# One attention and MLP kernel: the first score in two halves of its queries, head B's first row values by products with a unit matrix, and another order of the first two pairs

## What is computed

```python
# q, k, v: (4 batches, 8 heads, 576 positions, 64), f32
q_rot, k_rot = (rotate(q), rotate(k))          # [x1 cos - x2 sin, x1 sin + x2 cos]
scores = scale * np.matmul(q_rot, k_rot.transpose(0, 1, 3, 2))
scores = scores - np.max(scores, axis=-1, keepdims=True)
attn = np.exp(scores)
attn = attn / (np.sum(attn, axis=-1, keepdims=True) + 1e-09)
attn_out = np.matmul(attn, v)
# then, on the 2304 x 512 result: h = x @ w_in; solu = h * softmax(h);
# layer norm without bias times g_ln; @ w_out
```

## Time and profile before

| what | value |
|---|---|
| median of 3 runs | 488.84 us (488.19 to 488.97) |
| the profiled execution | 488.11 us, with a span of 486.3 us |
| granted TensorE clock | 1.00 of full speed |
| first maximum of pair 0 on PE | 11.29 us |
| first score of pair 0, of pair 1, of pair 2 | 16.13, 35.02, 52.46 us |

### The profile page before, as it was taken

How to read it: one execution, slowest core, us unless ns; L and a number is a source line. 1 busy time by engine, 2 the same in 40 slices (tenths; PEclk the granted TensorE clock), 3 DMA queues, 4 the chain that set the end, 5 groups by cost and what they waited for, 6 DMA issues and landing times.

```text
span 486.3 us, 7544 instructions
## 1 busy us (share of the span) xinstructions
PE 479.3 (99%) x2499; PEld 402.9 (83%) x2499; DVE 362.5 (75%) x566; ACT 255.3 (52%) x383; POOL 178.6 (37%) x208
## 2 busy tenths in 40 slices
PE   8899999999999999999999999999999999999997
PEld 8677888888888888888888878888888888888885
DVE  6767776787778678767866456999897899888731
ACT  4667777777677778777776353033223222322221
POOL 6855246426434642554361012343343121122110
PEclk9999999999999999999999999999999999999999
DMA  8503544545454544545423112233333233322232
GB/s 296 184 10 75 152 145 126 168 125 168 102 158 144 156 132 127 168 111 171 138 74 98 33 39 46 40 66 85 85 68 83 40 62 66 82 55 59 61 76 86
DMA packets 101006, 50.57 MB, mean 104 GB/s; under 512 B 90280, under 2 KB 90280, under 8 KB 99048
## 3 DMA queue, kind: packets, MB, share of 16 engines
q1 hardware_dynamic: 100152, 50.00, 38.1%
q10 hardware_dynamic: 816, 0.10, 0.1%
HBM read 33.33 MB, written 4.79 MB: 78 GB/s over the span
## 4 chain that ended last, share of the span: by engine, by line
PE 95%; DVE 2%; ACT 1%; DMA 1%; issue 0%; SPq 0%; DVEq 0%; ACTq 0%
PE ps L1022 25%; PE ps L1036 20%; PE ps L1050 20%; PE ps L989 18%; PE ps L960 8%; PE ps L1004 4%; DMA X<-x_in 1%; DVE X L681 1%; DVE nm L740 0%; ACT p_main L553 0%; DVE X L686 0%; ACT QK L509 0%; ACT QK L524 0%; DVE QK L715 0%; DVE KB L725 0%
## 5 line engine op out<-in xcount | busy, mean ns | idle before, releaser
L740 DVE TENSOR_REDUCE nm<-ps 128x1 fp32r<-128x576 f32 x144 | 108.0, 755 | 56.0 <-PE ps L960 54.0
L1022 PE MATMUL ps<-p_main,V 128*128 128x288 f32 x512 | 145.3, 406 | 0.0
L553 ACT ACTIVATE p_main<-ps 128x576 f32<-128x576 f32 x128 | 83.2, 650 | 47.0 <-PE ps L989 45.5
L1022 PEld LDWEIGHTS ps<-p_main,V 128*128 128x128 f32 x512 | 90.0, 190 | 13.7 <-ACT p_main L553 0.2
L381 POOL TENSOR_TENSOR X<-X,rope 128x1152 f32<-128x1152 f32 x26 | 68.3, 2643 | 89.2 <-DVE w_lo L757 89.0
L989 PE MATMUL ps<-QK 128*128 128x288 f32 x320 | 95.7, 380 | 0.8 <-ACT p_main L553 0.5
L1036 PE MATMUL ps<-w_hi,KB 128*128 128x512 f32 x288 | 91.5, 390 | 0.0
L1050 PE MATMUL ps<-w_hi,QK 128*128 128x512 f32 x288 | 91.0, 389 | 0.0
L989 PEld LDWEIGHTS ps<-QK 128*128 128x128 f32 x320 | 57.6, 189 | 20.8 <-issue 5.7
L989 PE MATMUL ps<-KB 128*128 128x288 f32 x320 | 67.8, 293 | 0.0
L574 ACT ACTIVATE X<-ps,neg_max 128x1024 f32<-128x1024 f32 x18 | 20.1, 1118 | 83.4 <-DVE neg_max L778 83.4
(11 more groups left out here) (88 smaller groups left out, 580.2 us busy)
## 6 DMA issues: line engine op xcount, KB each, us to landing
X<-x_in SPq DMA_DIRECT2D x13, 1152.0 KB, 5.1
V<-oe SPq DMA_DIRECT2D x213, 32.0 KB, 1.9
V<-v_in SPq DMA_DIRECT2D x32, 160.0 KB, 2.7
out<-X SPq DMA_DIRECT2D x18, 256.0 KB, 2.3
w_raw<-w_in SPq DMA_DIRECT2D x16, 256.0 KB, 2.9
xT<-x_in SPq DMA_DIRECT2D x2, 1152.0 KB, 10.3
xT<-oe SPq DMA_DIRECT2D x16, 144.0 KB, 2.4
inv<-inv_rows SPq DMA_DIRECT2D x16, 144.0 KB, 2.9
```

The costliest lines, as they stand in the source:

```text
L553: nc.scalar.activation(dst[:, :].rearrange("p (b c) -> p b c", b=2), score_ps[:, :, 0:HALF], ACT.Exp, scale=SCALE).then_inc(exp_done, 1)
L740: nc.vector.tensor_reduce(nm[g][:, at:at + 1], src[:, :, 0:HALF], AX_XY, ALU.max, negate=True)\
L1022: ins = nc.tensor.matmul(o_ps[a][:, half, 0:HALF], v, p[:, half * HALF:(half + 1) * HALF], start=(k == 0), stop=(k == 9))
```

## The change

Four things are edited:

- `score(0, 0)` and `score(0, 1)` are replaced by `half_score(s, half)`, each for 288 of the queries. The exponential of score 0 is taken in two instructions, one for each half. Row values 0 to 2 (`FRONT`) are copied to `KB` first, and the first half score stands ahead of the last row product.
- Head B's row values of pair 0 come from four products with the unit matrix (`first_row_b`) and one copy on ACT; DVE's transposition and SP's four DMAs for them go.
- The maxima of pair 1 begin at step 4 of pair 0 (before: step 3), those of pair 2 at step 1 of pair 1 (before: step 0), and `max_slot` gives the last six of pair 1 the banks 4, 5 and 0, 1 in turn.
- ACT's and DVE's work for pairs 1 and 2 is written at other steps; the second copy of pair 1's queries of head A moves from ACT (`second_queries(1, 0)`) to DVE.

```diff
-FIRST_MAXIMA = [((), (), ()), ((), (), ()), ((), (), ()), ((), (), (0,)), ((1,), (), (2,)), ((3,), (), (4,)),
-                ((), (5,), ()), ((6,), (), (7,)), ((), (8,), ())]
-SECOND_MAXIMA = [((), (), (0,)), ((), (1,), ())] + [((s,), (), ()) for s in range(2, STEPS)]
+FIRST_MAXIMA = [((), (), ())] * 4 + [((), (), (0,)), ((1,), (), (2,)), ((3,), (4,), ()), ((5,), (), (6,)), ((7,), (), (8,))]
+SECOND_MAXIMA = [((), (), ()), ((0,), (), (1,)), ((), (2,), ())] + [((s,), (), ()) for s in range(3, STEPS)]
...
-            if k < STEPS + SPARE:
-                return max_ps[2 * ((k - STEPS) % 2)], k - 1
+            if STEPS + SPARE <= k < 2 * STEPS:
+                return max_ps[(k - STEPS) % 2], k - 1
             return max_ps[0], k
...
-            sp.wait_ge(kb_ones[0], 2)
-            rows_of_b(0)
...
             act.wait_ge(kb_ones[0], 2)
-            act.wait_ge(first_rows, BOTH)
-            nc.scalar.activation(KB[0][D:D + 1, 1, 0:MAIN], ps[0:1, 2, 0:MAIN], ACT.Copy).then_inc(first_rows_set, 1)
+            act.wait_ge(first_rows, FRONT)
+            nc.scalar.activation(KB[0][D:D + 1, 1, 0:FRONT * P], ps[0:1, 3, 0:FRONT * P], ACT.Copy).then_inc(first_rows_set, 1)
             act.wait_ge(first_rows, BOTH + 1)
...
+            act.wait_ge(half_scored, 1)
+            nc.scalar.activation(p_main[0][:, 0:HALF], score_ps[:, 0, 0:HALF], ACT.Exp, scale=SCALE).then_inc(half_done, 1)
+            act.wait_ge(score_ready, 1)
+            nc.scalar.activation(p_main[0][:, HALF:S], score_ps[:, 1, 0:HALF], ACT.Exp, scale=SCALE).then_inc(exp_done, 1)
...
                         if s == 2:
+                            act.wait_ge(first_rows_b, BOTH)
+                            nc.scalar.activation(KB[0][0:1, 1, S + 2 * TAIL:WIDE], ps[0:1, 0, 0:MAIN], ACT.Copy)\
+                              .then_inc(first_rows_b_set, 1)
+                        if s == 3:
                             high(1, 0)
-                            second_queries(1, 0)
...
+            dve.wait_ge(rot_done, 2)
+            nc.vector.tensor_copy(QK[1][other(0), 0, 0:S], x_of(1)[own(0), 1, :]).then_inc(second_set, 1)
             low_keys(1, 0)
...
-                if s == 5:
-                    third_keys()
-                if s == 6:
-                    third_queries()
+                    if s == 7 and place == 0:
+                        third_keys()
+                        third_queries()
...
+            def first_row_b(j):
+
+                pe.wait_ge(max_taken, max(BOTH + j + 2, STEPS - 2))
+                nc.tensor.matmul(ps[0:1, 0, j * P:j * P + P], nm[1][:, j:j + 1], ident_r[:, :], start=True, stop=True)\
+                  .then_inc(first_rows_b, 1)
...
+            def half_score(s, half):
+
+                for k, (keys, queries) in enumerate(((QK[0][:, 1, :], QK[0][:, 0, :]), (KB[0][:, 0, :], KB[0][:, 1, :]))):
+                    ins = nc.tensor.matmul(score_ps[:, half, 0:HALF], keys[:, s * P:s * P + P],
+                                           queries[:, half * HALF:(half + 1) * HALF], start=(k == 0), stop=(k == 1))
+                return ins
...
             for i in range(3):
                 row_scores(0, i)
-            for j in range(BOTH):
+            for j in range(FRONT):
                 first_row(j)
                 row_scores(0, j + 3)
+            first_row(FRONT)
+            row_scores(0, STEPS - 3)
+            pe.wait_ge(low_q_done[0], 1)
+            pe.wait_ge(copy_done[0], 1)
+            pe.wait_ge(kb_ones[0], 2)
+            half_score(0, 0).then_inc(half_scored, 1)
             first_row(BOTH)
+            pe.wait_ge(first_rows_set, 3)
+            half_score(0, 1).then_inc(score_ready, 1)
             row_scores(0, STEPS - 2)
+            pe.wait_ge(half_done, 1)
+            half_score(1, 0)
+            row_scores(0, STEPS - 1)
+            pe.wait_ge(exp_done, 1)
+            half_score(1, 1).then_inc(score_ready, 1)
```

More of the change, by code:

```diff
@@ L231, in max_slot, with hi_set @@
                 return max_ps[k % 3], k - 2
-            if k < STEPS + SPARE:
-                return max_ps[2 * ((k - STEPS) % 2)], k - 1
+            if STEPS + SPARE <= k < 2 * STEPS:
+                return max_ps[(k - STEPS) % 2], k - 1
             return max_ps[0], k
+        def hi_set(m, a, copies):
+            by_vector = a == 0 and (m >= 2 or (m == 1 and copies == 2))
+            return 2 * m + copies - int(by_vector)
         def fronts(t):
@@ L610, in _ @@
                 for s in range(STEPS):
[L611 to L615, removed]
+                    if n or s:
+                        exp(n, s)
                     if n == 0:
                         if s == 2:
+                            act.wait_ge(first_rows_b, BOTH)
+                            nc.scalar.activation(KB[0][0:1, 1, S + 2 * TAIL:WIDE], ps[0:1, 0, 0:MAIN], ACT.Copy)\
+                              .then_inc(first_rows_b_set, 1)
+                        if s == 3:
                             high(1, 0)
-                            second_queries(1, 0)
-                        if s == 3:
+                        if s == 4:
                             high(1, 1)
-                        if s == 4:
+                        if s == 5:
                             second_queries(1, 1)
@@ L628, in _ @@
                             act.wait_ge(gain_loaded, 16)
+                        if s == 8:
+                            high(2, 0)
+                    elif n == 1:
+                        if s == 0:
+                            second_queries(2, 0)
+                        if s == 1:
+                            high(2, 1)
+                        if s == 2:
+                            take_o(0, 1)
+                        if s == 3:
+                            second_queries(2, 1)
+                        if s == 4:
+                            add_eps(0)
+                            w_high(0)
                     else:
-                        if s == 0 and 2 <= n < PAIRS - 1:
+                        if s == 0 and n < PAIRS - 1:
                             second_queries(n + 1, 1)
@@ L733, in row_max @@
                     dve.wait_ge(first_rows, BOTH + 1)
+                if i == BOTH + 1 and m == 1:
+                    dve.wait_ge(first_rows_b, BOTH)
                 if i == 0 and m >= 2:
                     dve.wait_ge(turned[0], m - 1)
-                if i == BOTH + 1 and m >= 1:
-                    dve.wait_ge(turned[1], m)
+                if i == BOTH + 1 and m >= 2:
+                    dve.wait_ge(turned[1], m - 1)
                 src = max_slot(k)[0]
@@ L741, in row_max @@
                   .then_inc(max_taken, 1)
-                if (i == BOTH and m >= 1) or i == STEPS - 1:
+                if m >= 1 and (i == BOTH or i == STEPS - 1):
                     dve.wait_ge(max_taken, k + 1)
@@ L947, in row_scores @@
                     pe.wait_ge(max_taken, ahead)
+                if k == STEPS:
+                    pe.wait_ge(first_rows_b_set, 1)
+                if k == STEPS + SPARE:
+                    pe.wait_ge(o_taken, 1)
                 if i == BOTH and m >= 1:
@@ L1084, in _ @@
                         weigh(of, k, 1)
+                    if n == 0 and s == 1:
+                        for j in range(BOTH):
+                            first_row_b(j)
                     for i in maxima(n, s)[2]:
```

66 lines of the change are left out of this document (42 added, 24 removed).

## The result

The changed kernel takes 490.28 us in the median (489.81 to 490.46, 7 runs), the kernel before 488.55 (7 runs, 0.3 us under the median of the first three). The ratio is 1.0033, with a 95% interval of 1.0023 to 1.0043: 1.7 us slower. Forecast was 488.7, no change. Two executions far longer than the rest, one of e7 (2759 us) and one of e8 (602 us), are left out of the ratios, and since the latter was e8's profiled one, at a granted clock of 0.754, no landmarks of e8 are given.

The account below looks back on a forecast made before the run. PE bounds the kernel, its chain covering 95% of the span. +0.2 us up to pair 1's first score and -0.3 in pair 1 give -0.1: 488.11 becomes 488.0, plus 0.73 to the median, 488.7; range 487.6 to 489.7.

Parts of the forecast that it names:

- Step 6: Pair 1: 10.8 us from its first score to its tails, -0.3 us; behind the tails the order of before.
- Step 5: Pair 0's tails to score 0 of pair 1: rows and POOL's low part ready at 35.1, score at 35.2, +0.2 us.
- Rival B: Slower, 489.3: pair 1's rows land 2.05 us after the last issue, score 0 of pair 1 at 36.0; chance 0.2.
- Step 2: Pair 0: maxima 7 and 8 come later behind the second half score; first product with V at 18.93, before 18.30.
- Steps 3 and 4: Pair 0: head B's four row products take 0.24 us, ACT's copy costs nothing; new turns start the tails at 26.86, before 27.51.
- Rival A: Faster, 487.6: the 0.6 us at the first V product and pair 1's two gates (0.6) are absent; chance 0.2.
- rival C: Slower, 490: POOL's late chain in pair 0 shifts maximum 4, the transposition and score 0 of pair 1 by 1 us; chance 0.1.

Follow-up runs that it names:

- e7: Kernel before with only head B's row values of pair 0 by four products and a copy on ACT; 489.46 us, ratio 1.0016.
- e8: Kernel before with pair 1's second head A query copy on DVE and two alternating slots for pair 1's maxima 5 to 8; 487.97 us, ratio 0.9988.
- e2: Kernel before with only ACT's two copies of pair 2's keys moved from steps 2 and 3 of pair 1 to 5 and 7; 489.03 us, ratio 1.0012.
- e1: Changed kernel with ACT's two copies of pair 2's keys back at steps 2 and 3 of pair 1; 489.80 us, ratio 1.0034.
- e3: As e1, with the first score and its exponential whole again and PE's order of before up to it; 488.79 us, ratio 1.0005.
- e6: Kernel before with only the first score and its exponential in halves; 489.63 us, ratio 1.0022.
- e4: As e1, with head B's rows of pair 0 again by DVE's transposition and SP's four DMAs; 489.34 us, ratio 1.0019.
- e10: Changed kernel with halves, row products and late key copies undone, and POOL's rotation of pair 3 not waiting for DVE's low part; 490.96 us, ratio 1.0047.

## Why the prediction was wrong

Forecast was -0.1 us at score 0 of pair 2, measured +1.85. By the table of landmarks:

- **Step 6, "Behind the tails the order is that of before": 0.75 us.** That is the step that failed, and not in a size. PE's list is the same there, ACT's isn't: the two key copies had moved into it. I counted PE's waits in pair 1 up to its tails and took the rest from PE's order alone. e2 shows the copies' price by themselves, 0.75, with the same starts as in the changed kernel. Behind them stands a second thing that the step left out: without the copies e1 gets back 0.45 and keeps 0.30, which is DVE and POOL being 0.3 us later against the tails: DVE's last low part of pair 2 ends 3.8 us ahead of the tails of pair 1 (43.99 and 47.77), before 4.1 (42.01 and 46.09).
- **Step 5, the rows' landing: 0.4.** The place and the gate were right, to the step from tails to transposition (4.14 us, forecast and measured). The landing was taken at the lower of its two bounds, 1.1 us from the start of the last issue; it is 1.45. That issue starts 3.10 us behind the transposition (32.21 to 35.31), not 2.93, and the score is 4.59 us behind it instead of 4.2. Rival B named this wait with the upper bound of 2.05; so it was the right mechanism, half as large. Its 489.3 for the kernel was closer than the forecast, but it too had nothing for the rest of the loss. The rule of the Trainium skill (DMA: Bandwidth & Descriptors, Anatomy of one DMA — SWDGE (gpsimd) path), about 2.0 us on the path through GpSimd, is above the 1.45 that this transfer took from SBUF to SBUF on SP's queue; the direction in which it spoke was right.
- **Step 2: 0.3.** Its mechanism is shown by e3 and e6, with 0.92 us at the first product with V, where 0.63 was forecast. Maximum 8 starts at 18.80 (18.13 and one step of 0.67) and is given on at 18.80 + 0.81 = 19.61, 0.1 later than drawn. From there to 19.80 PE has nothing to wait for that the program asks for. The cause of these 0.2 us stays open; in e4 the same gap is 0.4.
- **Steps 3 and 4: 0.08 and 0.26.** The products with the unit matrix take 0.11 each and not 0.06, between the bounds I had, but the first of them starts 0.84 us behind the product with V and not 0.97. Score 4 comes 1.64 us behind score 3, not 1.54, and the tails start 0.46 us behind the last maximum ahead of them, not 0.27 (27.61 and 28.07 in the changed kernel's timeline); before it was 0.46 too (27.05 and 27.51), which the walk passed over.
- **Step 6 up to the tails: 0.17**, 10.97 us for 10.8. Together 0.75 + 0.4 + 0.3 + 0.34 + 0.17 = 1.96 us, for the 1.95 between -0.1 and +1.85.

All of these terms err on the same side. Every start in the walk was the earliest that rows allow, so nearly every miss makes the kernel slower than forecast. The chance of slower by over 0.2% was given as 0.14, and the range ended at 489.7. What was right: that the halves gain nothing for the first exponential (it ends at 18.27 - 11.87 = 6.40, before at 17.61 - 11.29 = 6.32), that the new turns win time up to pair 0's tails, and that little of it is left at pair 1. Rival A (faster) found nothing; rival C's time of 490 is the one that came out, but by luck: its late POOL was not seen in pair 0, POOL's low keys of pair 1 end at 30.35, 0.5 us ahead of their use.

## What to carry to other kernels

Where one engine is full, list for every engine what has moved into each stretch, not only the full engine's own order: here two copies of 0.68 us each cost 0.75 us together at steps 5 and 7, and taking them away from steps 2 and 3 won nothing there (10.97 us up to the tails, in e1 10.98). Splitting a step so that its first part can start early brings nothing if the part's consumer stands in an in-order queue behind the same late work, and the pieces put into the full engine's queue ahead of other work delay that work. A gain is worth only as much as the next gate leaves: here 1.3 us at pair 0's tails came down to 0.04, by owed work, two gates within 0.3 us, and a later one. And a wait that seems to set only the order may keep two engines off each other.

## What the runs showed of the hardware

- DVE's subtraction of two SBUF tensors (64 x 576, f32) takes 0.75 us alone and 2.4 to 3.1 us when POOL's product of two SBUF tensors (128 x 1152) is under way; in e10 the second one ends at 45.39, 0.61 us behind POOL's pair of products (44.78), and the first at 42.29, some 0.6 behind the end of POOL's first product, which took its usual 2.65. POOL's second product takes 3.15 us there. So it looks less like running slowly than like waiting, on both engines in turn. DVE's reductions from PSUM keep their 0.76. The Trainium skill (SBUF — State Buffer, SBUF: two separate sides) describes it: the port pair that DVE and GpSimd share is held for a whole instruction, and an instruction of DVE with two SBUF inputs needs it against one of GpSimd that reads SBUF. The trace agrees.
- A DMA of 256 bytes (two pieces of 128) from SBUF to one partition's row took 1.45 us from issue to landing on SP's queue (35.31 to 36.76), and six issues in a row 3.3 us (32.45 to 35.8 with the last), so the last of six small DMAs lands 4.3 us after the first issue starts.
